# Attention, soft mixture and projection in one kernel: three seams between stages put in another order

## What is computed

```python
# attention: B=4, H=8, S=576, D=64, causal window 128, a linear bias per head
scores = q @ k.T / sqrt(D) + bias;  masked outside 0 <= i - j < 128
attn = exp(scores - max) / (sum + 1e-9);  out = attn @ v
x = out as [N=2304, 512]

# soft mixture: 8 experts with 4 slots each, w1 [8, 512, 1024], w2 [8, 1024, 512]
logits = x @ phi                       # [2304, 32]
d = softmax over the 2304 rows;        slot_input = d.T @ x
slot_out[e] = relu(slot_input[e] @ w1[e]) @ w2[e]
c = softmax over the 32 slots;         x = c @ slot_out

# projection: w_in [512, 2048], w_out [2048, 512]
h = x @ w_in;  g = h * clip(h + 3, 0, 6) / 6;  out = g @ w_out
```

## Time and profile before

| | |
|---|---|
| median of 3 runs | 451.46 us (451.17 to 452.02) |
| profiled execution | 451.76 us, its span 450.0 us |
| TensorE (PE) busy | 417.5 us, 93% of the span |
| VectorE (DVE) busy | 233.7 us, 52% |
| ScalarE (ACT) busy | 212.7 us, 47% |
| GpSimd (POOL) busy | 70.1 us, 16% |
| HBM | 135 GB/s over the span |
| mean granted TensorE clock | 0.976 |

### The profile page before, as it was taken

One profiled execution on the slowest core, in us unless ns is written; L12 is line 12 of the kernel. 1 busy time (PEld: TensorE's weight loads), 2 busy tenths in 40 slices (PEclk: granted clock), 3 DMA queues, 4 the chain that ended last, 5 costly groups with the idle time before them and its releaser, 6 DMA issues.

```text
span 450.0 us, 10183 instructions
## 1 busy us (share of the span) xinstructions
PE 417.5 (93%) x3764; PEld 341.0 (76%) x3764; DVE 233.7 (52%) x698; ACT 212.7 (47%) x601; POOL 70.1 (16%) x112
## 2 busy tenths in 40 slices
PE   3899999999999958887697999999999999999996
PEld 2688888878888844567475888888888888888885
DVE  2466686777678756040345534444354434454442
ACT  2788776878787710000635434343333434343431
POOL 1133133223223302000656000000000000000000
PEclk9999999999999986998998999999999999999999
DMA  9759898898797482999910100001010101010101
GB/s 179 190 149 259 225 260 218 236 260 230 202 286 189 132 311 86 387 386 396 396 55 1 40 7 23 25 0 47 0 47 0 47 0 47 0 47 0 47 1 48
DMA packets 75494, 61.41 MB, mean 136 GB/s; under 512 B 57792, under 2 KB 57792, under 8 KB 75456
## 3 DMA queue, kind: packets, MB, share of 16 engines
q1 hardware_dynamic: 75456, 60.89, 44.9%
HBM read 56.16 MB, written 4.72 MB: 135 GB/s over the span
## 4 chain that ended last, share of the span: by engine, by line
PE 86%; DVE 5%; ACT 4%; issue 3%; DMA 1%; SPq 0%; DVEq 0%
PE probs_turned L958 23%; PE out_turned L958 22%; PE scores L757 7%; PE probs_turned L766 4%; PE scores L901 4%; PE out_turned L782 4%; PE scores L940 4%; PE scores L886 3%; PE routes L812 3%; PE out_turned L786 3%; PE turns L740 2%; PE turns L797 2%; ACT probs L397 2%; PE turns L732 2%; PE routes L836 1%
## 5 line engine op out<-in xcount | busy, mean ns | idle before, releaser
L683 DVE SCALAR_TENSOR_TENSOR g<-u,scores 128x512 f32<-128x512 f32 x72 | 49.5, 688 | 109.7 <-ACT u L435 109.7
L440 ACT ACTIVATE g_hi<-g 128x512 fp32r<-128x512 f32 x72 | 45.5, 632 | 119.8 <-PE out_turned L958 119.1
L397 ACT ACTIVATE probs<-probs,rowmin 128x128 f32<-128x128 f32 (+1 forms) x160 | 62.0, 391 | 3.5 <-DVE rowmin L508 3.5
L958 PE MATMUL probs_turned<-w_out_hi,g_hi 128*128 128x512 f32 x144 | 57.5, 399 | 5.4 <-ACT g_hi L440 5.0
L958 PE MATMUL probs_turned<-w_out_lo,g_hi 128*128 128x512 f32 x144 | 57.1, 396 | 0.0
L958 PE MATMUL out_turned<-w_out_hi,g_hi 128*128 128x512 f32 x144 | 57.0, 396 | 0.0
L958 PE MATMUL out_turned<-w_out_lo,g_hi 128*128 128x512 f32 x144 | 56.9, 395 | 0.0
L958 PE MATMUL out_turned<-w_out_hi,g_lo 128*128 128x512 f32 x144 | 56.8, 394 | 0.0
L958 PE MATMUL probs_turned<-w_out_hi,g_lo 128*128 128x512 f32 x144 | 56.6, 393 | 0.0
L689 DVE TENSOR_TENSOR g_lo<-g,g_hi 128x512 fp32r<-128x512 f32 x72 | 53.1, 738 | 1.9 <-ACT g_hi L440 1.9
L435 ACT ACTIVATE u<-scores 128x512 f32<-128x512 f32 x72 | 41.9, 582 | 2.1 <-PE scores L940 2.1
(11 more groups left out here) (131 smaller groups left out, 627.2 us busy)
## 6 DMA issues: line engine op xcount, KB each, us to landing
weight_ring<-in_moe_w_dram SPq DMA_DIRECT2D x32, 1024.0 KB, 7.5
out_dram<-y SPq DMA_DIRECT2D x18, 256.0 KB, 2.0
q_in<-in_q_dram SPq DMA_DIRECT2D x16, 256.0 KB, 4.3
k_in<-in_k_dram SPq DMA_DIRECT2D x16, 256.0 KB, 4.6
v_in<-in_v_dram SPq DMA_DIRECT2D x16, 256.0 KB, 3.8
weight_ring<-in_moe_w_in_dram SPq DMA_DIRECT2D x8, 512.0 KB, 12.4
weight_ring<-in_moe_w_out_dram SPq DMA_DIRECT2D x4, 1024.0 KB, 15.5
q_in<-in_q_dram SPq DMA_DIRECT2D x4, 128.0 KB, 4.0
```

Of the source, the lines that this page charges most:

```text
L397: act.activation(probs[0:R, m % 2, h, :], probs[0:R, m % 2, h, :], ACT.Exp, bias=rowmin[0:R, m % 2, h:h + 1], scale=-1.0, accum_out=rsum[0 ...
L440: act.activation(g_hi[:, p % 2, :], g_sb[:, p % 4, :], ACT.Copy).then_inc(ghi_ready, 1)
L683: dve.scalar_tensor_tensor(out=g_sb[:, p % 4, :], in0=u_sb[:, p % 2, :], scalar=6.0, in1=bank[p % 4], op0=ALU.min, op1=ALU.mult).then_inc( ...
L958: ins = pe.matmul(bank[4 + kk][:, :], g[:, p % 2, cols], w[:, c, :], start=(p == 0 and i == 0 and a == 0), stop=(p == FPAIRS - 1 and i == ...
```

## The change

It has three parts.

- **Start.** q and k get semaphores of their own. The k of tiles 0 and 1 is transposed into `ps_b`, so its transposes don't wait for the copy of q; from tile 2 on they wait for both k's transfer and that copy. The scores of unit 1 move from step 1 to step 0, ahead of turn_q(1).
- **Last tile and slots.** In step 41 attend(39) moves ahead of turn_o(18) and route(18). In step 43 route(19) moves ahead of turn_o(19), and route has a wait for `ot_copied` in every tile. VectorE's normalise is split into `invert` (the reciprocals) and `normalise`, and for the last tile the second comes after `slot_part`. The transpose reads `acc` itself; the division by the slot sums is done in the instruction of the ReLU (the sums are positive), and the two operations for the reciprocal follow the copy to `slot_masked`.
- **Projection.** In unit 3 of the first chunk VectorE does low(3) ahead of gate(4).

```diff
@@ -101,7 +101,6 @@
     slot_m = place("slot_masked", [P, E * (KC * SLOTS + SPE)], tail + 17536)
     pick = place("pick", [P, QUADS, 6, SLOTS], tail + 17536, f32r)
     comb4 = place("combine4", [P, 2, TILES, 2, 2, SLOTS], tail + 21760)
-    slot_in = place("slot_in", [P, P], tail + 26880)
     so = place("slot_out", [P, P], tail + 26880)
     hid = place("hid", [P, CHUNK], tail + 27392)
     so_t = place("slot_out_t", [P, KC, SLOTS], tail + 27392)
@@ -132,7 +131,7 @@
         ps_u = ps_b[:, 0:HEADS * SLOTS]
         ps_col = ps_b[:, 256:256 + P + 1]
 
-        qk_in = [sem("qk_in0"), sem("qk_in1")]
+        q_ld, k_ld = [sem("q_in0"), sem("q_in1")], [sem("k_in0"), sem("k_in1")]
         vv_in = [sem(f"v_in{i}") for i in range(VRING)]
         phi_zeroed, phi_in = sem("phi_zeroed"), sem("phi_in")
         ring_in = [sem(f"ring_in{i}") for i in range(RING)]
@@ -157,7 +156,7 @@
         slots_summed, acc_done = sem("slots_summed"), sem("acc_done")
         late_zeroed = sem("late_zeroed")
         dve_step, comb_step = sem("dve_step"), sem("comb_step")
-        slot_scaled, slot_turned = sem("slot_scaled"), sem("slot_turned")
+        slot_turned = sem("slot_turned")
         slot_ready, ring_used = sem("slot_ready"), sem("ring_used")
         row_shifted, row_softened = sem("row_shifted"), sem("row_softened")
         comb_ready, comb_turned, comb_copied = sem("comb_ready"), sem("comb_turned"), sem("comb_copied")
@@ -174,6 +173,10 @@
 
         block = ctx.enter_context(nc.Block())
 
+        def k_bank(n):
+
+            return ps_b if n < 2 else ps_a
+
         def rows_of(n):
             return ROWS[n % TILES]
 
@@ -228,9 +231,9 @@
             def load_qk(n):
                 b, t = divmod(n, TILES)
                 wait(sp, k_turned, n - 1)
-                for src, dst in ((q, q_in), (k, k_in)):
+                for src, dst, landed in ((q, q_in, q_ld), (k, k_in, k_ld)):
                     sp.dma_start(dst[0:ROWS[t], n % 2, :, :], src[b, :, t * P:t * P + ROWS[t], :].rearrange(
-                        "h p d -> p h d")).then_inc(qk_in[n % 2], 16)
+                        "h p d -> p h d")).then_inc(landed[n % 2], 16)
 
             def load_v(n):
                 b, t = divmod(n, TILES)
@@ -372,7 +375,7 @@
                 act.wait_ge(k_turned, n + 1)
                 wait(act, scored, 2 * (n - KRING + 2) if n >= KRING else 0)
                 R = rows_of(n)
-                act.activation(k_t[:, n % KRING, :, 0:R], ps_a[:, :].rearrange("p (a m) -> p a m", m=P)[:, :, 0:R],
+                act.activation(k_t[:, n % KRING, :, 0:R], k_bank(n)[:, :].rearrange("p (a m) -> p a m", m=P)[:, :, 0:R],
                                ACT.Copy).then_inc(k_copied, 1)
 
             def copy_out(n):
@@ -511,13 +514,16 @@
                                              op0=ALU.add, op1=ALU.min,
                                              accum_out=rowmin[0:R, m % 2, h:h + 1]).then_inc(masked, 1)
 
-            def normalise(n):
+            def invert(n):
                 R = rows_of(n)
                 dve.wait_ge(exped, HEADS * (n + 1))
                 dve.tensor_scalar(rinv[0:R, 0, :], rsum[0:R, n % 4, :], 1e-9, None, ALU.add).then_inc(norm_step, 1)
                 dve.wait_ge(norm_step, 2 * n + 1)
                 dve.reciprocal(rinv[0:R, 1, :], rinv[0:R, 0, :]).then_inc(norm_step, 1)
                 dve.wait_ge(norm_step, 2 * n + 2)
+
+            def normalise(n):
+                R = rows_of(n)
                 if n >= XRING:
                     dve.wait_ge(slots_summed, (n - XRING) // TILES + 1)
                 dve.wait_ge(o_turned, n + 1)
@@ -583,10 +589,14 @@
                 if m == 4:
                     dve.wait_ge(consts, BATCHES + 4)
                 if output_in(m) is not None:
-                    normalise(output_in(m))
+                    invert(output_in(m))
+                    if output_in(m) < NT - 1:
+                        normalise(output_in(m))
                     route(output_in(m))
                 if batch_at(m, PART_AT) is not None:
                     slot_part(batch_at(m, PART_AT))
+                if output_in(m) == NT - 1:
+                    normalise(NT - 1)
                 if batch_at(m, SHIFT_AT) is not None:
                     slot_shift(batch_at(m, SHIFT_AT))
                 if batch_at(m, ACC_AT) is not None:
@@ -599,11 +609,6 @@
                 ins.then_inc(dve_step, 1)
                 dve.wait_ge(dve_step, counted[0])
 
-            dve.wait_ge(acc_done, BATCHES)
-            link(dve.tensor_scalar(rtot[:, :], acc[:, P:P + 1], 1e-9, None, ALU.add))
-            link(dve.reciprocal(rtot[:, :], rtot[:, :]))
-            dve.tensor_scalar(slot_in[:, :], acc[:, 0:P], rtot[:, 0:1], None, ALU.mult).then_inc(slot_scaled, 1)
-
             def own_slots(m, chunks, first, count):
 
                 width = chunks * SLOTS + SPE
@@ -614,6 +619,11 @@
             dve.wait_ge(late_zeroed, 1)
             dve.tensor_copy(own_slots(slot_m, KC, 0, KC), bank[3][:, 0:P].rearrange(
                 "p (c e s) -> p e c s", c=KC, s=SPE)).then_inc(slot_ready, 1)
+
+
+            dve.wait_ge(acc_done, BATCHES)
+            link(dve.tensor_scalar(rtot[:, :], acc[:, P:P + 1], 1e-9, None, ALU.add))
+            link(dve.reciprocal(rtot[:, :], rtot[:, :]))
 
 
             link(dve.tensor_reduce(rmax[:, 0, :], logits[:, :, :], AX.X, ALU.max))
@@ -646,7 +656,7 @@
             split_combine(0)
             split_combine(1)
             dve.wait_ge(ring_used, E)
-            dve.tensor_scalar(hid[:, :], bank[0][:, 0:CHUNK], 0.0, None, ALU.max).then_inc(hid_relu, 1)
+            dve.tensor_scalar(hid[:, :], bank[0][:, 0:CHUNK], rtot[:, 0:1], 0.0, ALU.mult, ALU.max).then_inc(hid_relu, 1)
             dve.wait_ge(hid_turned, 1)
             dve.wait_ge(late_zeroed, 2)
 
@@ -704,11 +714,12 @@
                         split_compact(1)
                     if isinstance(m, int) and n == 3:
                         copy_wp(2)
-                    if start:
+                    ahead = start or (isinstance(m, int) and n == 3)
+                    if ahead:
                         low(n, p)
                     if not (last and p == FPAIRS - 1):
                         gate(n + 1, (p + 1) % FPAIRS)
-                    if not start:
+                    if not ahead:
                         low(n, p)
                     if p == 0 and not (isinstance(m, int) and m == 0):
                         out_rows(m - 1)
@@ -726,7 +737,7 @@
         def _(pe):
             def turn_q(n):
                 R = rows_of(n)
-                pe.wait_ge(qk_in[n % 2], 32 * (n // 2 + 1))
+                pe.wait_ge(q_ld[n % 2], 16 * (n // 2 + 1))
                 wait(pe, normed, n - 3)
                 for a in range(PAIRS):
                     ins = pe.transpose(ps_a[:, a * P:a * P + R], q_in[0:R, n % 2, 2 * a:2 * a + 2, :].rearrange(
@@ -735,9 +746,11 @@
 
             def turn_k(n):
                 R = rows_of(n)
-                pe.wait_ge(q_copied, n + 1)
+                pe.wait_ge(k_ld[n % 2], 16 * (n // 2 + 1))
+                if n >= 2:
+                    pe.wait_ge(q_copied, n + 1)
                 for a in range(PAIRS):
-                    ins = pe.transpose(ps_a[:, a * P:a * P + R], k_in[0:R, n % 2, 2 * a:2 * a + 2, :].rearrange(
+                    ins = pe.transpose(k_bank(n)[:, a * P:a * P + R], k_in[0:R, n % 2, 2 * a:2 * a + 2, :].rearrange(
                         "p h d -> p (h d)"), ident[0:R, 0:R])
                 ins.then_inc(k_turned, 1)
 
@@ -799,6 +812,7 @@
 
             def route(n, m):
                 R = rows_of(n)
+                pe.wait_ge(ot_copied, n + 1)
                 wait(pe, logit_done, n)
                 if n == 0:
                     pe.wait_ge(phi_in, 32)
@@ -842,7 +856,10 @@
             turn_q(0)
             turn_k(0)
             for m in range(LAST):
-                if m < UNITS:
+                if m == 0:
+                    scores(0)
+                    scores(1)
+                elif 2 <= m < UNITS:
                     scores(m)
                 if 1 <= m <= UNITS:
                     turn_probs(m - 1)
@@ -852,10 +869,15 @@
                     sum_slots(batch_at(m, SUM_AT))
                 if turns_in(m) is not None:
                     turn_q(turns_in(m))
-                if output_in(m) is not None:
+                if m == UNITS + 1:
+                    attend(m - 2)
+                if output_in(m) == NT - 1:
+                    route(NT - 1, m)
+                    turn_o(NT - 1)
+                elif output_in(m) is not None:
                     turn_o(output_in(m))
                     route(output_in(m), m)
-                if 2 <= m <= UNITS + 1:
+                if 2 <= m <= UNITS:
                     attend(m - 2)
                 if batch_at(m, CMAX_AT) is not None:
                     turn_max(batch_at(m, CMAX_AT))
@@ -874,8 +896,8 @@
 
             slot_view = slot_m[:, 0:E * KC * SLOTS].rearrange("p (e c s) -> p e c s", e=E, s=SLOTS)
```

(4 more changed lines are left out.)

## The result

The changed kernel takes 449.88 us in the median of 20 runs, the one before 451.36 in 20 runs beside them: 1.5 us less. The ratio of the means is 0.995, 95% interval 0.9936 to 0.9965, so 2.2 us faster (1.6 to 2.9). One of the 20 runs, 527.75 us at a mean granted clock of 0.744, is left out of the ratio; without it the median is 449.61. Measured once more, beside the third set of experiments, the changed kernel took 450.93 against 451.37, ratio 0.9986 (0.9967 to 1.0005). The forecast was 446.8 and a range up to 449.3: the direction is right, and less than half of the gain arrived.

A forecast was written before the change was run, and what follows sets the result against it. The prediction took TensorE to bound attention and the steady final projection, so only seams between stages pay. Its terms, 1.3 + 0.8 - 0.8 + 3.5 = 4.8 us saved, gave 446.8 us, range 445.3 to 449.3.

The forecast's parts named there:

- Seam 1: Start of attention: first transposes and scores wait less, so attention runs 1.3 us earlier, bounds 0.5 to 1.9.
- a longer attention: Named sign of a wrong forecast: attention longer by more than 1 us between its first and last scores.
- The added waits: 38 fulfilled TensorE waits: free in attention, but shifting instruction-stream stops in the expert stage; 0.8 us lost.
- one more stop of 2.49: Expert stage: upper bound on the added waits' loss, one more full TensorE stop of 2.49 us.
- All points then come a little earlier: Expert stage: stops reached 15 matmuls sooner let work resume 0.4 us earlier, the last ready near 214.6.
- Seam 2 (a): Last attention tile: attend(39) ahead of turn_o(18) and route(18) changes nothing, the same work lying before the copy.
- (b): Last tile: route(19) ahead of turn_o(19), normalising after the column maximum; gains 0.15 us, bounds -0.2 to 0.5.
- Seam 2 (c): Slots: transposing acc directly brings the copy to slot_masked 0.62 us sooner, then limited by GpSimd's memset.
- it is passed on: Handover to experts: the last-tile-and-slots gain of 0.8 us also makes the weight stream start 0.8 earlier.
- Seam 3: Projection's first chunk: low(3) ahead of gate(4) gains 3.5 us, bounds 1.3 to 3.9, no clock fall.
- one more whole stop: Rival in the expert stage: added waits cost a full stop, 2.49 instead of 0.8; 448.5 us, chance 0.08.
- small seam 3: Rival in the projection: gain only 1.3, as low(4) waits for GpSimd and the clock falls; 449.0 us, chance 0.13.

The follow-up runs named there:

- the third set of experiments: Follow-up runs on the last tile's order, the clock and the cause of the stops, beside the kernel before at 451.37 us.
- w29_waits: Kernel before with only the 38 added TensorE waits in turn_k and route: 454.37 us, ratio 1.007 to the kernel before.
- a0_all_no_waits: Kernel before plus all three parts, without the added TensorE waits except route's in the last tile: 447.34 us, ratio 0.99.
- f1_trim_full: Kernel before plus start, low part and whole last-tile-and-slots part, with implied TensorE waits dropped: 446.29 us, ratio 0.9891.
- s2_slots: Kernel before plus only the last-tile-and-slots part, with its 20 added waits: 453.46 us, ratio 1.0052.
- f2_trim_route: As f1_trim_full, but attend(39) stays behind route(18), against the kernel before: 445.68 us, ratio 0.9873.
- t13_no_waits: Kernel before plus the start and the low part only, without added instructions: 445.94 us, ratio 0.9878.
- t13b_relu: As t13_no_waits, with the slot division also moved to the ReLU, against the kernel before: 446.16 us, ratio 0.9877.

## Why the prediction was wrong

- **Seam 1, right.** turn_q(0) at 4.22 (forecast 4.15), scores(0) at 7.17 (7.26), turn_probs(0) 1.70 sooner (1.2), and 1.41 at the last scores call (1.3). The order of the waits was read well from the rows. The sign of wrong that was named, a longer attention, didn't come.
- **The added waits, mis-sized.** This is the term that failed: "I take 0.8 lost", bound by one more stop of 2.49. The mechanism was right, and nearly the place: a fourth block boundary was put 15 matmuls before the stage's end and fell 11 before it. By itself it costs 3.2 us (w29_waits), in the whole change 2.3 to 3.9 by the ratios (0.99 in a0_all_no_waits; 0.995 and 0.9986 for the changed kernel). The step that failed is "All points then come a little earlier" by 0.4. The starts are set by packets 6.2 to 6.5 us apart, and a boundary that is reached 15 matmuls sooner waits for the same packet: counted from the first matmul with w2, work started again at 6.11, 12.57 and 18.76 before, at 6.04, 12.50, 18.79 and 24.98 in the changed kernel, and at 6.48, 12.94, 19.23 and 25.43 in w29_waits. The earlier stops grew instead (the one near 196 from 0.13 in the chain of before to 1.07), and the stage was 1.48 longer in the changed kernel, 1.93 in w29_waits. Left out altogether was the clock: with the last stop 5 or 11 matmuls before the end, `compact` ran mostly at the 1.2 GHz level in all four such traces and took 3.08 to 3.48 instead of 1.98, 1.23 more in the changed kernel. Together that is 2.71 in its trace, above even the bound of 2.49. In the table the two are 1.48 of the 2.09 and the 1.23; 0.53 of the 2.09 is the w1 stage, which was slower by the clock. 1.60 came back later, because the first project call ran at the high clock, which it had not before. By the six and seven traces above that is chance and no gain of the change.
- **Seam 2 (a) and (b), wrong in sign.** "the same work lies before it either way: nothing" was said of (a). For (b) "VectorE also gets tile 18 later by the length of attend(39)" was written down, and priced as part of a small gain. What was missed is that route(19) waits for `logit_done` of tile 18. In the old order turn_o(19) and the copy of o_t covered that wait; with attend(39) ahead and nothing in between it is 1.22. By the traces the step loses 0.3 where the clock fell later (f1_trim_full, s2_slots), and up to 1.6 where it fell at route(18). Without (a), route(19) doesn't wait for the logits, and (b) gains 0.4 (f2_trim_route), near the upper end of what was forecast.
- **Seam 2 (c), right in place and in its limit.** The memset is what is late next, and the gain is 0.53 (0.62 by its rows; the sum took 0.65). But "it is passed on" is not shown in time: t13_no_waits and t13b_relu take the same.
- **Seam 3, right.** low(3) before gate(4) for 0.69, project(3) without a wait, a pause of 1.20 (forecast 1.3), no fall of the clock; low(4), with GpSimd busy beside it, took 1.00: 3.33 in the table and 3.6 alone, against 3.5.
- **The sum.** 1.41 + 0.53 + 3.33 + 0.51 = 5.8 gained, 1.56 lost in the last tile, and 1.7 net in the expert stages and their clock (2.09 + 1.23 - 1.60). The rival "one more whole stop" with 448.5, at a chance of 0.08, had the right mechanism. The small seam 3 with 449.0 lies nearer in number, but its seam came in full. Had the 1.60 not come back, the profiled execution would have been that much further off.

Open are three points: what makes the clock fall or stay behind the same stop; whether the early fall of the clock in the new order has a cause in it, or is chance (by 161.2 in three of five traces, in none of eight of the old order), and whether the 0.5 us of the later division would show in time over more runs.

## What to carry to other kernels

Under a full DMA a short-matmul stage on TensorE can be bound by the arrival of its instructions; then each instruction added ahead of it moves the points where it stops, and the place of the last one can decide more than a hidden wait saves. So look at the queue of instruction packets beside the chain, don't add waits that another implies (38 of them, 29 instructions, cost 3.2 us), and count a schedule's instructions as one counts its microseconds. When a call is moved, go through every wait of what now stands behind it, and ask which call had covered it before. Taking out still more waits moved the stops as expected, but no gain in time is shown for it.

## What the runs showed that was not expected

- Fulfilled waits showed no price in their own place (last scores call at 153.84 against 153.61, with nearly all of the 38 ahead of it), and cost 3.2 us in all through the place of the stops, 40 us later.
- The stops' size goes with the DMA: 2.50 us at about 386 to 400 GB/s, 0.30 at 53 GB/s, with the same instructions. Each start follows a 16 KB packet of the instruction queue by 2.4 to 2.6 us.
- In a stage of 256 matmuls with few of them per microsecond (w1, 15 to 17 us) the length varied by 1.6 us between kernels with the same instructions there (15.31 to 16.88), by how long the clock stayed at 1.2 GHz after the idle chain ahead of it (2.5 us and 5.7 us, by the mean granted clock).
